# Logit rows turned and summed by VectorE, chunks loaded without k by token, and another order of the SW stage

## The reference

```python
# 1. retention attention, 8 heads of 64
state = gamma * state + k_t^T v_t;   y_t = scale * q_t @ state
x = y.transpose(0, 2, 1, 3).reshape(3072, 512)
# 2. soft mixture: 8 experts x 4 slots = 32 slots, w1 (8, 512, 1024), w2 (8, 1024, 512)
logits = x @ phi                                   # (3072, 32)
d = softmax(logits, axis=0);  slot_input = d.T @ x
slot_out = relu(slot_input[e] @ w1[e]) @ w2[e]     # per expert
x = softmax(logits, axis=1) @ slot_out
# 3. top-2 mixture: w1b (8, 512, 1024), w2b (8, 1024, 512)
noisy = x @ w_gate + log1p(exp(x @ w_noise)) * noise
top2 of noisy per token, weights softmax over the two
out[token] += weight * relu(x[token] @ w1b[e]) @ w2b[e]
```

## Time and profile before

| | |
|---|---|
| median of three runs | 538.63 us (537.22 to 539.7) |
| profiled execution | 540.1 us |
| its span, first to last instruction | 538.3 us |
| TensorE, VectorE, ScalarE, GpSimd busy | 92%, 51%, 34%, 47% of the span |
| mean granted TensorE clock | 0.974 |
| chain that ended last | TensorE 83%, DMA 9%, issue 2%, VectorE 2%, ScalarE 1% |
| DMA engines' busy share in tenths, 40 slices of 13.5 us | 8999999998999999444465342132232332423410 |
| moved from HBM and to it | 93.87 MB and 29.43 MB |

### The profile page before, as it was taken

How to read it: one execution, slowest core, us unless ns; L and a number is a source line. 1 busy time by engine, 2 the same in 40 slices (tenths; PEclk the granted TensorE clock), 3 DMA queues, 4 the chain that set the end, 5 groups by cost and what they waited for, 6 DMA issues and landing times.

```text
span 538.3 us, 13565 instructions
## 1 busy us (share of the span) xinstructions
PE 496.1 (92%) x4844; PEld 294.9 (55%) x4845; DVE 274.6 (51%) x443; ACT 185.5 (34%) x346; POOL 255.3 (47%) x217
## 2 busy tenths in 40 slices
PE   4998999997987568999999999999999999999995
PEld 3877787873577234444544544545545445445452
DVE  2674767575230796564646455464545332433422
ACT  0221222221003636846445363554442222223210
POOL 1221222212000013475777878786878766666553
PEclk9998999998997888999999999999999999999998
DMA  8999999998999999444465342132232332423410
GB/s 274 393 338 408 367 377 409 396 382 300 387 424 427 384 413 392 161 133 141 168 215 196 97 145 49 24 60 46 42 61 42 53 48 43 59 40 42 60 21 2
DMA packets 35096, 107.93 MB, mean 201 GB/s; under 512 B 11871, under 2 KB 13135, under 8 KB 32624
## 3 DMA queue, kind: packets, MB, share of 16 engines
q1 hardware_dynamic: 20880, 92.90, 44.8%
q0 software_dynamic: 14176, 14.49, 14.3%
HBM read 93.87 MB, written 29.43 MB: 229 GB/s over the span
## 4 chain that ended last, share of the span: by engine, by line
PE 83%; DMA 9%; issue 2%; DVE 2%; ACT 1%; SPq 1%; POOL 1%; DVEq 0%; POOLq 0%
PE ps L1022 51%; PE ps L1005 5%; PE ps L675 4%; PE ps L739 4%; DMA w_region<-moe_w 4%; DMA late_w1a<-chunks 3%; PE ps L888 3%; PE ps L859 3%; DMA w_region<-chunks 2%; PE ps L931 2%; PE ps L715 2%; PE ps L729 2%; PE ps L750 1%; PE ps L689 1%; PE ps L771 1%
## 5 line engine op out<-in xcount | busy, mean ns | idle before, releaser
L1022 PE MATMUL ps<-w_region,s_region 128*128 (+1 forms) x1304 | 290.3, 379 | 0.3 <-issue 0.3
L1022 PEld LDWEIGHTS ps<-w_region,s_region 128*128 128x128 f16 x1304 | 125.4, 98 | 141.5 <-issue 0.4
L1676 DVE SCALAR_TENSOR_TENSOR s_region<-ps,s_region 128x1024 f16<-128x1024 f32 x55 | 67.3, 1224 | 141.3 <-ACT s_region L1235 141.2
L1235 ACT ACTIVATE s_region<-ps 128x1024 f16<-128x1024 f32 x55 | 56.3, 1024 | 178.7 <-PE ps L1005 174.3
L625 POOL DMA_INDIRECT out<-s_region,rec_region x42 | 67.9, 1617 | 18.6 <-issue 11.6
L619 POOL DMA_INDIRECT out<-s_region,rec_region x41 | 54.9, 1339 | 37.2 <-DVE s_region L1706 32.6
L613 POOL DMA_INDIRECT rec_region<-records,idx x55 | 59.9, 1090 | 22.9 <-issue 16.4
L559 POOL TENSOR_TENSOR s_region<-w_region,s_region 128x512 f32<-128x512 f32 x14 | 14.6, 1043 | 51.7 <-PE ps L750 37.0
L1005 PEld LDWEIGHTS ps<-s_region,sw_region 128*128 (+1 forms) x440 | 29.6, 98 | 14.4 <-issue 1.2
L1706 DVE TENSOR_SCALAR s_region<-ps,rec_region,y_scale 128x512 f32<-128x512 f32 x42 | 33.8, 804 | 5.8 <-PE ps L1022 4.1
L1005 PE MATMUL ps<-s_region,sw_region 128*128 128x128 f16 x440 | 34.6, 219 | 0.6 <-ACT s_region L1230 0.4
(11 more groups left out here) (249 smaller groups left out, 576.0 us busy)
## 6 DMA issues: line engine op xcount, KB each, us to landing
w_region<-moe_w SPq DMA_DIRECT2D x49, 512.0 KB, 11.2
w_region<-moe_w SPq DMA_DIRECT2D x10, 2048.0 KB, 9.7
w_region<-chunks SPq DMA_DIRECT2D x26, 512.0 KB, 7.0
s_region<-moe_w SPq DMA_DIRECT2D x4, 2048.0 KB, 13.0
sw_region<-chunks SPq DMA_DIRECT2D x12, 512.0 KB, 7.2
late_w1a<-chunks SPq DMA_DIRECT2D x8, 512.0 KB, 7.6
w_region<-moe_w SPq DMA_DIRECT2D x3, 1024.0 KB, 8.3
s_region<-moe_w SPq DMA_DIRECT2D x5, 512.0 KB, 8.3
```

The source lines that it names most:

```text
L1022: last = nc.tensor.matmul(bank[6 + r], h[:, r, f, :], w2b_parts[:, bass.ds(o, 1), part, f, :].rearrange("p e m -> p (e m)"), start=(first ...
L1235: nc.scalar.activation(h_hi[:, r, :, :].rearrange("p c t -> p (c t)").rearrange("p (a n) -> p a n", a=2), ps[:, 2 + 2 * r:4 + 2 * r, :], A ...
L1676: nc.vector.scalar_tensor_tensor(out=h_lo[:, r, :, :].rearrange("p c t -> p (c t)").rearrange("p (a n) -> p a n", a=2), in0=ps[:, 2 + 2 * ...
```

## The change

1. `load_qk` loads only turned q (256 KB) for the last chunk of each batch.
2. The logit rows are no longer multiplied by `stack`. TensorE turns the 128 x 128 partial logits (`nc.tensor.transpose`), and VectorE adds the four groups of 32 with a `tensor_reduce` out of PSUM. `keep_logits` leaves ScalarE's list; in VectorE's it stands at the head of each chunk for t-2, and the last two are added behind the last chunk. The turned rows share their place with the turned maxima.
3. The groups of the SW stage become experts 0 to 3, 4 and 5, 6 and 7. Experts 4 and 5 are scaled, split and spread before `sw_product(7)`, around `hidden_b(0)`; 6 and 7 follow together behind six of the eight second `first_rows`. `sw_out[7]` moves to the bank of `sw_out[6]`, so product(7) waits for sums(6).
4. The spreads go round banks 6, 1, 0, 7 for eight units and then 1, 0, 7; the first two combines are turned in bank 6.
5. ScalarE's and VectorE's lists follow this order. `w2b_low(0)` is cut in two and moves behind the lows of 4 and 5.

```diff
--- before.py
+++ after.py
@@ -369,13 +369,13 @@
 
         block = ctx.enter_context(nc.Block())
 
-        SW_GROUPS = ((0, 4), (4, E - 1), (E - 1, E))
-        SW_BANKS = (6, 1, 0, 7, 6, 1, 0, 6, 6, 1, 7, 6, 1, 7, 0, 1)
+        SW_GROUPS = ((0, 4), (4, 6), (6, E))
+        SW_BANKS = (6, 1, 0, 7, 6, 1, 0, 7, 1, 0, 7, 1, 0, 7, 1, 0)
         SW_BY_DVE = (9, 11, 13, 15)
         SW_BY_ACT = tuple(u for u in range(2 * E) if u not in SW_BY_DVE)
         W2B_SUMS = 2
         FINE = 3
-        sw_out = [ps[:, 2 + e // 2, e % 2 * QF:(e % 2 + 1) * QF] for e in range(E - 1)] + [ps[:, 0, 0:QF]]
+        sw_out = [ps[:, 2 + e // 2, e % 2 * QF:(e % 2 + 1) * QF] for e in range(E)]
         SC = ((0, 1), (2, 3))
         Y, T_X, ST = 4, 6, 7
         y_of = [bank[Y + i][:, 0:2 * P] for i in range(2)]
@@ -383,9 +383,8 @@
         parts_at = bank[Y + 1][:, 2 * P:3 * P]
         den_at = bank[Y + 1][:, 400:402]
         state_at = bank[ST][:, 0:NP * D]
-        rows_at = bank[ST][:, NP * D:NP * D + SL]
-        turned_at = bank[ST][:, NP * D + SL:NP * D + SL + P]
-        spread_at = bank[ST][:, NP * D + SL + P:NP * D + 2 * SL + P]
+        rows_at = turned_at = bank[ST][:, NP * D:NP * D + P]
+        spread_at = bank[ST][:, NP * D + P:NP * D + SL + P]
 
 
         def wait_consumed(engine, b, c):
@@ -442,7 +441,8 @@
             def load_qk(g):
                 if g >= QK_DEPTH:
                     wait_consumed(sp, (g - QK_DEPTH) // NC, (g - QK_DEPTH) % NC)
-                load_words(qk_in[g % QK_DEPTH], g, 2 * DM, qk_full[g % QK_DEPTH])
+                n = DM if g % NC == NC - 1 else 2 * DM
+                load_words(qk_in[g % QK_DEPTH][:, 0:n], g, 2 * DM, qk_full[g % QK_DEPTH])
 
             load_words(kv_in[0][:, 0:DM], 0, 0, turned_full)
             load_words(qk_in[0][:, 0:DM], 0, 2 * DM, turned_full)
@@ -701,7 +701,7 @@
                     pe.wait_ge(cols_shifted, g + 1)
                 if t > 0:
                     pe.wait_ge(logits_kept, t)
-                nc.tensor.matmul(rows_at, logit_parts[t % 2], stack, start=True, stop=True).then_inc(logits_done, 1)
+                nc.tensor.transpose(rows_at, logit_parts[t % 2], ident[:, :]).then_inc(logits_done, 1)
 
             def turn_x(t):
 
@@ -919,12 +919,9 @@
 
             def sw_product(e):
                 w = w1b_home[e].rearrange("p (c f) -> p c f", c=DC)
-                if e % 2 == 1 and e < E - 1:
+                if e % 2 == 1:
 
                     pe.wait_ge(sw_sum_ready, e)
-                if e == E - 1:
-
-                    pe.wait_ge(*sw_kept(6))
                 pe.wait_ge(w1b_full[e], 16 if e < FINE else 16 * REP)
                 for d in range(DC):
                     for j in range(REP):
@@ -938,10 +935,7 @@
                 for half in range(2):
                     unit = 2 * e + half
                     before_it = [u for u in range(unit) if SW_BANKS[u] == SW_BANKS[unit]]
-                    if unit == 10:
-
-                        pe.wait_ge(ct_ready, 2)
-                    elif before_it:
+                    if before_it:
 
                         pe.wait_ge(*sw_kept(before_it[-1]))
                     for j in range(2):
@@ -987,8 +981,9 @@
                 nc.tensor.transpose(bank[to][:, 0:P // 2].bitcast(F16), c_rows[:, r, :, :].rearrange("p n s -> p (n s)"),
                                     ident_h[:, :]).then_inc(ct_turned, 1)
 
-            pe.wait_ge(*sw_kept(3))
-            turn_c(0, 0, 7)
+            pe.wait_ge(*sw_kept(4))
+            turn_c(0, 0, 6)
+            sw_spread_parts(4)
 
             def code_of(i):
                 return pe.value_load(tile_code[0:1, bass.ds(i, 1)], min_val=0, max_val=E * E - 1)
@@ -1033,18 +1028,18 @@
                                      start=(part == 0 and f == 0), stop=False)
 
             hidden_b(0, 0, 0)
-            turn_c(1, 1, 7)
+            sw_spread_parts(5)
+            turn_c(1, 1, 6)
             sw_product(7)
-            pe.wait_ge(*sw_kept(7))
-            for e in range(4, 7):
-                sw_spread_parts(e)
-            pe.wait_ge(*sw_kept(11))
+            pe.wait_ge(ct_ready, 2)
             pe.wait_ge(w2b_hi_ready, 2)
             pe.wait_ge(h_hi_ready, 1)
             first_rows(0, range(FC))
+            pe.wait_ge(w2b_lo_ready, 1)
+            first_rows(1, range(FC - 2))
+            sw_spread_parts(6)
             sw_spread_parts(7)
-            pe.wait_ge(w2b_lo_ready, 1)
-            first_rows(1, range(FC))
+            first_rows(1, range(FC - 2, FC))
             pe.wait_ge(tile_code_ready, 1)
             pe.wait_ge(*sw_kept(14))
             pe.wait_ge(*sw_kept(15))
@@ -1088,10 +1083,6 @@
 
         @block.scalar
         def _(act):
-            def keep_logits(t):
-                act.wait_ge(logits_done, t + 1)
-                nc.scalar.activation(logits[:, t, :], rows_at, ACT.Copy).then_inc(logits_kept, 1)
-
             def keep_chunk(t):
                 act.wait_ge(parts_done, t + 1)
                 if t > 1:
@@ -1102,12 +1093,8 @@
                     if GROUPS[n][0] == t - len(x_ring):
 
                         act.wait_ge(slot_in_done, n + 1)
-                if t == NT - 1:
-                    keep_logits(t - 1)
                 act.wait_ge(x_turned, t + 1)
                 nc.scalar.activation(x_home(t), bank[T_X][:, :], ACT.Copy).then_inc(x_kept, 1)
-                if 0 < t < NT - 1:
-                    keep_logits(t - 1)
 
             def exp_slots(g):
                 act.wait_ge(cols_shifted, g + 1)
@@ -1126,7 +1113,6 @@
                     exp_slots(g)
                     if g < NG - 2:
                         keep_den(g)
-            keep_logits(NT - 1)
             exp_slots(NG - 1)
             keep_den(NG - 2)
             keep_den(NG - 1)
@@ -1213,10 +1199,8 @@
             act.wait_ge(sw_scale_ready, 1)
             for e in range(4):
                 sw_high(e)
-            sw_keep(0)
-            sw_keep(1)
             sw_sums(5)
-            for unit in range(2, E):
+            for unit in range(4):
                 sw_keep(unit)
 
             def stage_c(i, r, arrival):
@@ -1227,7 +1211,7 @@
 
             def keep_ct(i, r):
                 act.wait_ge(ct_turned, i + 1)
-                nc.scalar.activation(ct[:, r, :], bank[7 if isinstance(i, int) and i < 2 else r][:, 0:P // 2].bitcast(F16),
+                nc.scalar.activation(ct[:, r, :], bank[6 if isinstance(i, int) and i < 2 else r][:, 0:P // 2].bitcast(F16),
                                      ACT.Copy).then_inc(ct_ready, 1)
 
             def h_high(i, r):
@@ -1236,21 +1220,26 @@
                                      ps[:, 2 + 2 * r:4 + 2 * r, :], ACT.Relu).then_inc(h_hi_ready, 1)
 
 
+            act.wait_ge(sw_scale_ready, 2)
+            for e in range(4, 6):
+                sw_high(e)
+            sw_keep(4)
+            sw_keep(5)
+            stage_c(0, 0, rec_arrival(0))
+            sw_keep(6)
             sw_sums(6)
-            stage_c(0, 0, rec_arrival(0))
             keep_ct(0, 0)
+            sw_keep(7)
+            sw_keep(8)
+            h_high(0, 0)
             stage_c(1, 1, rec_arrival(1))
-            h_high(0, 0)
+            sw_keep(10)
             keep_ct(1, 1)
-            act.wait_ge(sw_scale_ready, 2)
-            for e in range(4, 7):
+            sw_sums(7)
+            act.wait_ge(sw_scale_ready, 3)
+            for e in range(6, E):
                 sw_high(e)
-            sw_sums(7)
-            sw_keep(8)
-            sw_keep(10)
             sw_keep(12)
-            act.wait_ge(sw_scale_ready, 3)
-            sw_high(7)
             sw_keep(14)
             stage_c(2, 0, rec_arrival(2))
             w2b_sums(EARLY, junk)
@@ -1320,6 +1309,11 @@
                 ins.then_inc(dve_step, 1)
                 dve.wait_ge(dve_step, steps[0])
 
+            def keep_logits(t):
+                dve.wait_ge(logits_done, t + 1)
+                nc.vector.tensor_reduce(logits[:, t, :], rows_at.rearrange("p (j s) -> p s j", j=REP), AX_X,
+                                        ALU.add).then_inc(logits_kept, 1)
+
             def find_max(g):
                 dve.wait_ge(logits_kept, GROUPS[g][1])
                 if g > 0:
@@ -1376,6 +1370,8 @@
             def sequence_copies(b):
                 for c in range(NC):
                     t = b * NC + c
+                    if t > 1:
+                        keep_logits(t - 2)
                     for g in group_ending(t - 1):
                         find_max(g)
                     keep_x_t(b, c)
@@ -1419,6 +1415,8 @@
                 return a.rearrange("p e t -> p t e")
 
 
+            keep_logits(NT - 2)
+            keep_logits(NT - 1)
             find_max(NG - 1)
             join_max(NG - 1)
             shift_cols(NG - 1)
@@ -1601,7 +1599,7 @@
                 power_scale(sw_scale, sw_sum[:, 1, first:last], slice(first, last), SW_TOP, sw_scale_ready)
 
             def sw_low(e):
-                dve.wait_ge(sw_hi_ready, e // 2 * 2 + 2 if e < 6 else e + 1)
```

(12 more changed lines are left out.)

## The result

The changed kernel took **536.55 us** (median of 20 runs, 533.26 to 541.61); the kernel before, run beside it 20 times, took 539.07 (536.1 to 541.1). The ratio is 0.9958 with an interval of 0.9941 to 0.9975: about 2.3 us faster, within 0.5%. The forecast was 537.2.

What follows compares the result with a forecast made beforehand. The steady TensorE loop from 225.87 us is untouched, so only its start counts, set by attention stretch, weight stretch and SW tail. 0.95 + 0.1 + 0.4 = 1.45 us off 538.63 gives 537.2 us; range 534.8 to 539.3.

Steps and rivals of the forecast that it cites:

- Term 0.95 us: Attention stretch: of 2.6 us cut from the load queue, TensorE can take 0.64 plus chunk 17's stall of 0.31.
- the walk: Prediction's step-by-step timing: load stalls at chunks 6, 7, 8 and 17; SW's four engine queues followed from product(5).
- The sign of a lower DMA share at the end: End of the attention stretch: DMA share in 119 to 123 us lower than 0.66 would show the forecast right.
- the step "that is 0" on TensorE: Logit rows: TensorE loses two 32-column matmuls (0.14 us) and gains one transpose (0.15 us), so no net change.
- the 0.1 I took: End of the last chunk: the new sum ends at 124.1 us, gaining 0.1 us; bounds -0.2 and 0.3.
- 0.4 us with product(7) on its landing: SW tail: the loop's start gains only unit 14's 0.3 to 0.5 us, taken as 0.4; product(7) no earlier relative to its load.
- That hidden(1) would be 1.3 us sooner: SW tail on TensorE: hidden(1) starts at 220.1 us instead of 221.4, most of it not reaching the loop's start.
- The step "this queue and the landing meet within 0.2 us": Ahead of product(7): turn_c(1), behind ScalarE's queue, ends at about 212.1 us; expert 7's w1b lands at 212.0.
- rival E: ScalarE's queue ahead of product(7) is longer than walked; product(7) 1.5 to 2 us behind its load, 539.0 us; chance 0.06.
- Rival B: More arrives: no stall or half clock near 42 us, hidden(1)'s 1.3 us also arrive; 3.2 us gained, 535.4; chance 0.20.
- C: Halved loads nearly as slow as whole ones, or the freed time idle: 0.6 us gained, 538.0 us; chance 0.12.
- D: VectorE becomes the bound of a chunk: up to 0.3 us in each of 24 chunks, 544.2 us; chance 0.04.

Runs made afterwards that it cites:

- after: Profiled execution of the changed kernel, set against that of the kernel before: 538.69 us, span 536.8 (before: 538.3).
- the changed kernel again: The changed kernel repeated unaltered beside its variants, against the kernel before: 537.14 against 536.41 us, ratio 1.0010 (0.9978 to 1.0043).
- three sums: Changed kernel with each VectorE logit sum made three times, two results unread: 539.69 us once, beside 538.92 of the kernel before.
- early read: Changed kernel with TensorE's read of tile 1's code moved to just behind product(7): 537.2 us once, beside 538.92 of the kernel before.
- the pool: All runs of the study together, across chips: median 537.6 us for the kernel before (102 runs), 536.6 for the changed kernel (32 runs).

## Why the prediction was right, and where not

**The halved loads: right, as far as the scatter lets one see.** Term 0.95 us. Alone they gave about 0.6 us in the medians, with an interval that touches no change. The price of one load is confirmed: a halved one lands 0.67 us behind its neighbour, a whole one 1.28 (0.64 to 0.67 and 1.34 in the prediction). The mechanism is seen too: chunk 8 was still stalled (1.61 us), and the wait of chunk 17 is missing in eight of ten traces. But the walk had no stall between chunks 8 and 17, and there are such: 0.52 us at chunk 16 in after, 0.73 and 0.53 at chunks 10 and 15 with the loads alone. They move from execution to execution and eat part of what was won. The marker at chunk 8 moved by 1.47 in after and by 1.80 with the loads alone, and not by the 0.64 of one half load. Of the 1.47 the halved load makes 0.67; the rest arose in loads that the diff does not touch, and kernels with whole loads are 0.5 to 1.4 us earlier there than before as well. The sign of a lower DMA share at the end means nothing, since before has the same idle time two microseconds later. The worry that a load of half the size saves no queue is out, by the two landings. The Trainium skill, "DMA: Bandwidth & Descriptors", Bandwidth, would by its 138 GB/s for small transfers have let the halving save nothing; the 0.67 us against 1.28 speak against that here.

**The logit rows: right in direction, the step "that is 0" on TensorE was mis-sized.** It is 0.03 us a chunk, 0.7 us in all. The end gained 0.3 us, the upper bound rather than the 0.1 I took. The sum on VectorE was 0.28 us where 0.3 was taken, and the idle time of 1.17 us covered it (0.94 left). The decay behind it kept its 0.84 us; the shared port pair of which the Trainium skill, "SBUF — State Buffer", "SBUF: two separate sides", tells did not show on a sum that reads PSUM. By the markers the part is worth about 1 us, not 0.1; the medians alone show 0.5.

**The order of SW: the tail as forecast, the gain not to be seen.** The prediction said 0.4 us with product(7) on its landing. Behind product(7) the tail became 0.35 us shorter against the kernel with the other two parts (13.03 to 12.68). The reason is the one that the prediction gave for its 0.4: the copy of combine 2 waits for the two w2b sums, and these start as soon as unit 14 is evicted, 0.35 us sooner. That hidden(1) would be 1.3 us sooner is wrong: it stands 8.7 us behind product(7) in the new order and 8.6 in both kernels with the old one and full clock there. It was only before's own execution that needed 9.3, and the prediction was made from that one. That hidden(1) then started at 220.10 in after, the very figure of the walk, is luck, for product(7) was earlier than walked and the tail behind it longer.

The step "this queue and the landing meet within 0.2 us" failed. Five traces have the new order of turn_c(1) and product(7) and a recorded landing. product(7) waited for the load in one of them (order alone, 0.13 us behind the landing) and stood behind ScalarE in the others: 0.44 us behind the landing (rows and order), 0.66 (the changed kernel again), 0.66 (three sums) and, with a stretch at half clock in the queue, 2.1 (early read). So rival E, to which the prediction gave a chance of 0.06, came in three of five by its own sign of over 0.5 us, though at full clock at about a third of its price. In after the landing itself is only partly recorded. It was not that the walk of ScalarE was too short: counted from the index of the tile order, the walk put product(7) at 11.9 us, and it came at 10.8 to 11.1 in after and in the two kernels nearest to it (rows and order; the changed kernel again). The landing is what the walk had wrong. It took the 11.8 us of before for fixed, and in the other traces the landing came 9.2 to 12.5 us behind the index, in most of them between 9.9 and 10.6. One part of the queue the walk did not have: ScalarE stood 0.59 us for the record of tile 0, which lands 5.4 to 6.3 us after its fetch is issued, and 0.37 and 0.43 us in those two. That is most of the 0.44 and 0.66 by which product(7) was late there. Net effect of part 3: no gain that can be measured (1.0000 alone; 1.6 and 1.7 us slower than without it in two comparisons that the scatter leaves open).

**The sum.** 0.95 + 0.1 + 0.4 = 1.45 was forecast; by the runs it is some 0.6 + 1.0 + 0, with each term uncertain by as much as itself. The total agrees better than its terms do, and that is partly luck: the pool gives 1.0 us, the first comparison 2.5, the repetition none. Rival B is not seen in after, since the half clock near 42 us stayed. In eight of the twelve later traces it was absent there, also in two kernels with whole loads and with stalls of 1.64 and 1.34 us at chunk 8. So it belongs to the execution and not to the change, and B's condition, that no stall is left, is not what decides it. Without it the scores of chunk 9 follow those of chunk 8 in 5.3 to 5.4 us instead of 6.7 to 6.8. C is refuted by the landings, D by the idle time that is left, also under three sums.

## What to carry to other kernels

When an engine's queue is reordered, walk it from the landing of each transfer that it needs, small fetches included: a combine that is moved up may find its record not there and carry that wait to whatever is behind it. And do not take a landing from one trace as fixed: here it moved by three microseconds against the step that it was to meet, so an order in which neither has to wait for the other is worth more than one in which both just meet. Count the passes and the weight loads of a matmul too, and price it by its own rows. And when a chain has two holders in a row, here a register read and a pair of sums on another engine, moving one alone shows nothing; move both, and only as far as the next stage has room. Last, a marker of one trace against one of another is no measurement: two executions of the changed kernel put product(7) at 211.40 and at 207.53 us.
